# Linear attention ahead of two feed-forward layers: state summed in PSUM, chunks in pairs, 64 by 64 products

## The reference

```python
gamma = 1.0 - 2.0 ** (-5.0 - np.arange(H))          # one decay per head
for t in range(S):
    state = gamma * state + outer(k[:, :, t], v[:, :, t])     # 64 x 64 per head
    y[:, :, t] = scale * (q[:, :, t] @ state)
x = y as (B * S, H * D)                              # 1536 x 512
x = gelu_like(x @ w_in) @ w_out                      # 512 -> 2048 -> 512
x = rms_normalised(x); out = (silu(x @ w_gate) * (x @ w_val)) @ w_out2    # 512 -> 1536 -> 512
```

## Time and profile before

| | us |
|---|---|
| median of 3 runs (586.87 to 587.15) | 587.14 |
| the profiled execution's own time | 587.46 |
| its span, first to last instruction | 585.6 |
| attention: first scores to first product of the layers | 5.46 to 55.26 |
| TensorE busy over the span | 575.1 (98%) |

### The profile page before, as it was taken

One profiled execution on the slowest core, in us unless ns is written; L12 is line 12 of the kernel. 1 busy time (PEld: TensorE's weight loads), 2 busy tenths in 40 slices (PEclk: granted clock), 3 DMA queues, 4 the chain that ended last, 5 costly groups with the idle time before them and its releaser, 6 DMA issues.

```text
span 585.6 us, 9221 instructions
## 1 busy us (share of the span) xinstructions
PE 575.1 (98%) x3558; PEld 552.0 (94%) x3558; DVE 356.0 (61%) x472; ACT 307.8 (53%) x533; POOL 169.2 (29%) x187
## 2 busy tenths in 40 slices
PE   6999999999999999999999999999999999999997
PEld 6888999999999999999999999998889999998886
DVE  3599555667334666876426768668764666667332
ACT  1556666744325766654337655563544555564321
POOL 2674444000122452000123453410060544420000
PEclk8999999999999999999999999999999999999999
DMA  8990122321211222322202222223213322223202
GB/s 324 347 315 29 58 69 72 109 86 59 73 37 36 73 73 72 109 73 72 67 8 72 73 73 73 72 73 108 73 37 103 114 72 73 73 72 109 72 0 107
DMA packets 24363, 52.83 MB, mean 90 GB/s; under 512 B 1920, under 2 KB 2048, under 8 KB 24320
## 3 DMA queue, kind: packets, MB, share of 16 engines
q1 hardware_dynamic: 23744, 50.93, 26.9%
q10 hardware_dynamic: 576, 1.32, 0.6%
HBM read 49.09 MB, written 3.15 MB: 89 GB/s over the span
## 4 chain that ended last, share of the span: by engine, by line
PE 95%; DVE 2%; DMA 2%; issue 1%; SPq 0%; ACT 0%
PE bank L470 39%; PE bank L420 17%; PE bank L422 17%; PE bank L423 17%; DMA arena<-attn_in 2%; PE bank L394 1%; PE bank L363 1%; PE bank L388 1%; DVE arena L823 1%; PE bank L373 1%; DVE arena L841 1%; PE bank L511 0%; DVE x_lo L723 0%; DVE w_lo L714 0%; DVE t L736 0%
## 5 line engine op out<-in xcount | busy, mean ns | idle before, releaser
L420 PE MATMUL bank<-x_hi,w_hi 128*128 128x384 f32 x560 | 187.3, 334 | 0.0
L423 PE MATMUL bank<-x_hi,w_lo 128*128 128x384 f32 x560 | 187.1, 334 | 0.0
L422 PE MATMUL bank<-x_lo,w_hi 128*128 128x384 f32 x560 | 187.1, 334 | 0.0
L714 DVE TENSOR_TENSOR w_lo<-raw,w_hi 128x512 fp32r<-128x512 f32 (+2 forms) x148 | 145.9, 1001 | 50.9 <-ACT w_hi L543 50.7
L975 POOL TENSOR_TENSOR raw<-raw 128x256 f32<-128x256 f32 x40 | 31.9, 796 | 324.1 <-DMA raw<-w 324.1
L543 ACT ACTIVATE w_hi<-raw 128x512 fp32r<-128x512 f32 (+2 forms) x148 | 109.0, 763 | 18.5 <-PE bank L423 10.2
L420 PEld LDWEIGHTS bank<-x_hi,w_hi 128*128 128x128 f32 x560 | 105.1, 188 | 0.1
L422 PEld LDWEIGHTS bank<-x_lo,w_hi 128*128 128x128 f32 x560 | 105.1, 188 | 0.1
L423 PEld LDWEIGHTS bank<-x_hi,w_lo 128*128 128x128 f32 x560 | 105.1, 188 | 0.0
L573 ACT ACTIVATE g_hi<-arena 128x768 fp32r<-128x768 f32 x56 | 47.5, 848 | 103.1 <-PE bank L470 103.1
L749 DVE TENSOR_TENSOR g_lo<-arena,g_hi 128x768 fp32r<-128x768 f32 x56 | 55.2, 986 | 75.2 <-ACT g_hi L573 75.2
(11 more groups left out here) (70 smaller groups left out, 591.0 us busy)
## 6 DMA issues: line engine op xcount, KB each, us to landing
raw<-w SPq DMA_DIRECT2D x68, 512.0 KB, 3.5
arena<-attn_in SPq DMA_DIRECT2D x22, 512.0 KB, 6.7
out<-x SPq DMA_DIRECT2D x1, 1536.0 KB, 7.8
out<-x SPq DMA_DIRECT2D x6, 256.0 KB, 2.0
arena<-attn_in ACTq DMA_DIRECT2D x2, 512.0 KB, 8.1
arena<-tables SPq DMA_DIRECT2D x1, 512.0 KB, 6.7
arena<-tables ACTq DMA_DIRECT2D x1, 256.0 KB, 10.6
ident<-ident_in SPq DMA_DIRECT2D x1, 64.0 KB, 11.4
```

Of the source, the lines that this page charges most:

```text
L420: pe.matmul(dst, w_hi[q][:, w], x_hi[:, x], start=start and kk == 0, stop=False, skip_group_check=True)
L422: pe.matmul(dst, w_hi[q][:, w], x_lo[:, x], start=False, stop=False, skip_group_check=True)
L423: mm = pe.matmul(dst, w_lo[q][:, w], x_hi[:, x], start=False, stop=kk == 1, skip_group_check=True)
L714: dve.tensor_tensor(w_lo[q % 3][:, dst], src, w_hi[q % 3][:, dst].bitcast(F32), ALU.subtract)\
```

## The change

1. **State in PSUM.** The recurrence "new = decay x old + contribution" is replaced by a running sum that is not decayed. The keys of chunk c are scaled by a table of their own, the old one times gamma to the power of -128c (`k_table`); the contributions of a batch are then summed by TensorE in one PSUM bank (`val[g]`, `start` only in chunk 0), and VectorE makes the state from the sum with one multiplication (`g_table`), or a copy for chunk 0. ScalarE's multiplications of the state (line 637) and the semaphore for them are gone.
2. **The tables** are worked out at the start. Two rows of the decay table are fetched by two new transfers, each copied to all 128 partitions (128 x 8 numbers), ahead of ScalarE's other transfers. VectorE multiplies them, GpSimd takes the power -1, VectorE refines it in three instructions, and makes four tables for keys and three for states, each instruction behind the one before it. The masks wait for the last of them.
3. **Compact state.** The state is 128 x 256, the zeros are gone, and so are the two memsets; the cross part is 8 products of 64 by 64 of the array in place of 4 of 128 by 128, both heads of a pair into the same bank, on different partitions.
4. **Pairs of chunks.** TensorE does the scores of two steps, the cross part of two, then contribution, outputs of both, contribution. VectorE, ScalarE, GpSimd and SyncE are ordered to match, and the preparations for the layers lie elsewhere.
5. **One mask instruction.** The PSUM banks of a step's scores are one tensor of 1024 columns (`twin`), multiplied by one instruction.
6. **Transfers.** SyncE loads queries and keys of step 1 ahead of the mask, and the first weights in the first batch of transfers.

Eleven small instructions stand ahead of the first mask, where before there were two memsets. The core of the diff:

```diff
-        state = [part(512) for _ in range(2)]
-        state_dec = [part(512) for _ in range(2)]
+        state = [part(256) for _ in range(2)]
+        k_table = [table[:, T_K:T_K + HEADS]] + [part(HEADS) for _ in range(1, CHUNKS - 1)]
+        g_table = [None, table[:, T_G:T_G + PAIRS]] + [part(PAIRS) for _ in range(2, CHUNKS - 1)]
...
             load(0)
+            load(1)
             sp.dma_start(table[:, T_MASK:T_Q], tables[:, T_MASK:T_Q]).then_inc(mask_in, 16)
-            load(1)
+            load_kv(2)
             load(2)
-            load_kv(2)
             load(3)
             load_kv(3)
+            load_weights(0)
...
+            for a in range(SLOTS, STEPS, 2):
+                for b in (a, a + 1):
+                    sp.wait_ge(scores_done, b - SLOTS + 1)
+                    if (b - SLOTS) % CHUNKS > 0:
+                        sp.wait_ge(q_decayed, cross_at(b - SLOTS) + 1)
+                    load(b)
+                for b in (a, a + 1):
+                    sp.wait_ge(y_done, b - SLOTS + 1)
+                    load_kv(b)
...
+            def new_products(a):
+                r, m = a % SLOTS, state_at(a)
+                g, c = chunk_of(a)
+                if c == CHUNKS - 1:
+                    return
...
+                pe.wait_ge(k_decayed, m + 1)
+                if c > 0:
+                    pe.wait_ge(state_done, m)
+                for p in range(PAIRS):
+                    for h in range(2):
+                        mm = pe.matmul(val[g][64 * h:64 * h + 64, cols(p, 64)],
+                                       k_dec[m % 2][:, cols(2 * p + h, 64)], v[:, cols(2 * p + h, 64)],
+                                       start=c == 0 and p == 0, stop=c == CHUNKS - 2, skip_group_check=True)
+                mm.then_inc(kv_done, 1)
+
+            def from_state(a):
+                par, x = a % 2, cross_at(a)
+                if a >= 2:
+                    pe.wait_ge(y_copied, a - 1)
+                if a % CHUNKS > 0:
+                    pe.wait_ge(q_decayed, x + 1)
+                    pe.wait_ge(state_done, x + 1)
                     for p in range(PAIRS):
-                        mm = pe.matmul(gate[par][:, cols(p, P)], state[x % 2][:, cols(p, P)],
-                                       q_dec[x % 2][:, cols(p, P)], start=p == 0, stop=False, skip_group_check=True)
+                        for h in range(2):
+                            rows = slice(64 * h, 64 * h + 64)
+                            mm = pe.matmul(gate[par][rows, cols(p, P)], state[x % 2][rows, cols(p, 64)],
+                                           q_dec[x % 2][rows, cols(p, P)], start=p == 0, stop=False,
+                                           skip_group_check=True)
                     mm.then_inc(cross_done, 1)
...
+            for a in range(0, STEPS, 2):
+                scores(a)
+                scores(a + 1)
+                if a == 0:
+                    new_products(0)
+                    from_state(0)
+                    from_chunk(0)
+                    from_state(1)
+                    new_products(1)
+                else:
+                    from_state(a)
+                    from_state(a + 1)
+                    new_products(a + 1)
+                    from_chunk(a)
+                from_chunk(a + 1)
+                if a + 2 < STEPS:
+                    new_products(a + 2)
...
+            for k, row in enumerate((first_row, next_row)):
+                at_ = (CHUNK - 2) * k
+                act.dma_start(row, tables[at_:at_ + 1, T_K:T_K + HEADS].to_broadcast([P, HEADS])).then_inc(rows_in, 16)
...
-                if c < CHUNKS - 2:
-                    act.wait_ge(state_done, m + 1)
-                    for p in range(PAIRS):
-                        ins = act.activation(state_dec[m % 2][:, cols(p, P)], state[m % 2][:, cols(p, P)],
-                                             ACT.Copy, scale=table[:, T_G + p:T_G + p + 1])
-                    ins.then_inc(state_decayed, 1)
...
+            dve.wait_ge(rows_in, 32)
+            dve.tensor_tensor(growth, first_row, next_row, ALU.mult).then_inc(decay_set, 1)
+            dve.wait_ge(inverted, 1)
...
+            for c in range(1, CHUNKS - 1):
+                dve.wait_ge(decay_set, c + 3)
+                dve.tensor_tensor(k_table[c], k_table[c - 1], power, ALU.mult).then_inc(decay_set, 1)
+            for c in range(2, CHUNKS - 1):
+                dve.wait_ge(decay_set, c + 6)
+                dve.tensor_tensor(g_table[c], g_table[c - 1], g_table[1], ALU.mult).then_inc(decay_set, 1)
...
+                dve.tensor_tensor(prob[a % 2], twin[a % 2][:, :], table[:, T_MASK:T_Q], ALU.mult)\
+                   .then_inc(probs_done, 1)
...
+                if c == 0:
+                    ins = dve.tensor_copy(state[m % 2], val[g][:, 0:256])
+                else:
+                    new, sums = (t.rearrange("p (k e) -> p k e", k=PAIRS) for t in (state[m % 2], val[g][:, 0:256]))
+                    ins = dve.tensor_tensor(new, sums, g_table[c].unsqueeze(2).to_broadcast([P, PAIRS, 64]), ALU.mult)
...
             dve.wait_ge(mask_in, 16)
+            dve.wait_ge(decay_set, 2 * CHUNKS - 1)
+            for a in range(0, STEPS, 2):
+                masked(a)
+                if a == 0:
+                    new_state(0)
+                masked(a + 1)
                 if a == 4:
                     lower_x(0, B11)
+                elif a == 8:
+                    sum_x(0, T2)
+                new_state(a + 1)
...
+            pool.tensor_tensor(power, growth, minus_one, ALU.pow).then_inc(inverted, 1)
             pool.wait_ge(decay_in, 16)
             decay_k(0)
-            decay_k(1)
             pool.wait_ge(q_table_in, 16)
+            pool.wait_ge(decay_set, 2 * CHUNKS - 1)
+            for a in range(0, STEPS, 2):
+                for b in (a, a + 1):
+                    if b % CHUNKS > 0:
+                        decay_q(b)
+                for b in (a + 1, a + 2):
+                    if b < STEPS and b % CHUNKS < CHUNKS - 1:
+                        decay_k(b)
```

More of the change, by code:

```diff
@@ L100, in transformer_kernel @@
         k_dec = [part(512) for _ in range(2)]
-        state = [part(512) for _ in range(2)]
-        state_dec = [part(512) for _ in range(2)]
+        state = [part(256) for _ in range(2)]
+        k_table = [table[:, T_K:T_K + HEADS]] + [part(HEADS) for _ in range(1, CHUNKS - 1)]
+        g_table = [None, table[:, T_G:T_G + PAIRS]] + [part(PAIRS) for _ in range(2, CHUNKS - 1)]
+        first_row, next_row = part(HEADS), part(HEADS)
+        growth, rest, power = part(HEADS), part(HEADS), part(HEADS)
+        minus_one = part(HEADS)
         used[0] = 0
@@ L107, in transformer_kernel @@
         m5 = [part(HALF) for _ in range(2)]
-        bank = [ctx.enter_context(nc.psum_tensor(f"bank{i}", [P, 512], F32)) for i in range(8)]
+        twin = [ctx.enter_context(nc.psum_tensor(f"twin{i}", [P, 1024], F32)) for i in range(2)]
+        bank = [twin[i // 2][:, 512 * (i % 2):512 * (i % 2) + 512] for i in range(4)]
+        bank += [ctx.enter_context(nc.psum_tensor(f"bank{i}", [P, 512], F32)) for i in range(4, 8)]
         acc, gate, val = bank[0:4], bank[4:6], bank[6:8]
@@ L352, in _, with scores @@
         def _(pe):
[L354 to L356 removed]
+            def scores(a):
+                par, r = a % 2, a % SLOTS
+                q, k = slot[r][:, 0:512], slot[r][:, 512:1024]
                 pe.wait_ge(qk_in[r], 16 * (a // SLOTS) + 16)
                 if a >= 2:
[L359 removed]
+                    pe.wait_ge(probs_done, a - 1)
                 for p in range(PAIRS):
@@ L396, in outputs @@
                                        prob[par][:, 512 * h + P * p:512 * h + P * p + P],
-                                       start=not cross and p == 0, stop=True, skip_group_check=True)
+                                       start=a % CHUNKS == 0 and p == 0, stop=True, skip_group_check=True)
                 mm.then_inc(y_done, 1)
@@ L625, in _, with copy_y @@
             act.wait_ge(decay_in, 16)
-            for a in range(STEPS):
-                par, m = a % 2, state_at(a)
+            def copy_y(a):
                 g, c = chunk_of(a)
@@ L832, in new_state @@
                     dve.wait_ge(cross_done, m - 1)
-                if c > 0:
-                    dve.wait_ge(state_decayed, (CHUNKS - 2) * g + c)
-                for h in range(2):
-                    rows = slice(64 * h, 64 * h + 64)
-                    new, old = (t[m_ % 2][rows, :].rearrange("p (k e) -> p k e", k=PAIRS)[:, :, 64 * h:64 * h + 64]
-                                for t, m_ in ((state, m), (state_dec, m - 1)))
-                    kv = val[m % 2][rows, 0:256].rearrange("p (k e) -> p k e", k=PAIRS)
-                    if c > 0:
-                        ins = dve.tensor_tensor(new, kv, old, ALU.add)
-                    else:
-                        ins = dve.tensor_copy(new, kv)
+                if c == 0:
[3 more added lines that the diff above has]
```

(1 more changed line is left out.)

125 lines of the change are left out of this document (50 added, 75 removed).

## The result

| | before | changed |
|---|---|---|
| median, us | 587.14 | 590.22 (589.81 to 590.75) |
| profiled execution's own time, span | 587.46, 585.6 | 590.75, 589.0 |
| ratio of the runs | | 1.0043, 95% interval 1.0028 to 1.0058 |
| first product of the layers | 55.26 | 57.39 |

Forecast were 585.2 and 581.8 to 588.2. In the profile the attention ends 2.1 us later than before, where I had it 1.9 us earlier, and 1.3 more are lost behind it: from the layers' first product to the end it is 531.6 us and was 530.3.

The account below looks back on a forecast made before the run. TensorE, busy 98% of the span, was taken as the bound; -3.9 us of shapes, -2.7 of waits and +4.7 at the start took the median from 587.14 to 585.2 us, range 581.8 to 588.2.

Parts of the forecast that it names:

- Tile shapes, -3.9 us: TensorE in the attention: groups of one kind side by side pay for fewer tile-shape changes, saving 3.9 us.
- 64 by 64 products, zero: Cross part: the two heads' products run side by side at the old pace, no gain and no loss.
- The small transfers, +4.4 us: Start, ScalarE's queue: two transfers of 128 small pieces delay what stands behind them by 2.2 us each, 4.4 together.
- the pace in the sum: Start: a small packet costs its queue a large one's time, queues taking turns; 117 packets in some 2.3 us.
- The 0.2 us worked out: Start: the skill page's 10.5 ns per small packet would have both small transfers gone in 0.2 us; not adopted.
- The half clock, 0 to 1.5, taken 0.5: Start: TensorE, mostly idle from 8.7 to 18, runs partly at 1.2 GHz, costing 0 to 1.5 us, 0.5 taken.
- Nothing, with the same cover: Slots in the pairs: step a+4's keys and values, needed 6.8 less 1.2 us after request, land in time; no cost.
- What is late next ... 2 us of slack: VectorE: pair 10's mask comes up to 0.5 us late behind pair 8's extras, but its output has 2 us slack.
- The waits of before, -2.7: Middle of the attention: TensorE's 2.7 us of waits, chiefly for states VectorE made late, go with the sum in PSUM.
- rival D: Slower: query table past 20 us, or middle pairs each waiting some tenths for GpSimd; 588 to 590, chance 0.08.
- the forecast 31.65 us of the pairs: TensorE's time for the five pairs from step 2 on, up to the layers: 31.65 us, including 2.75 for shapes.

Follow-up runs that it names:

- y2: y1 with TensorE's order alone changed to scores(a), cross(a), scores(a+1), cross(a+1) in pairs 2, 4, 8 and 10; 586.59 us, ratio 0.9963.
- x1: The kernel before with only the two small transfers added ahead of ScalarE's others, into a buffer nobody reads; 591.65 us, ratio 1.0055.
- z3: The changed kernel itself, unmodified, measured again in 9 runs beside the kernel before; 590.12 us, ratio 1.0032.
- x3: The changed kernel with 24 products of ones keeping TensorE busy in two waits of the start; 588.42 us, ratio 0.9999.
- x4: The changed kernel with six slots instead of four, so keys and values are asked for two outputs earlier; 588.09 us, ratio 0.9995.
- y1: The changed kernel without the small transfers and the power (factor by memsets), and with six slots; 585.14 us, ratio 0.9938.
- y4: The changed kernel with only VectorE's preparations reordered as in y3; ratio 1.0003.
- y3: y1 with VectorE's preparations for the layers in another order; 583.66 us, ratio 0.9917.
- z2: y3 with the mask moved ahead of step 1's queries and keys, the query table ahead of its keys and values; 582.80 us, ratio 0.9909.
- z1: y3 with 5 and 6 products of ones in TensorE's two waits of the start; 582.97 us, ratio 0.9913.

## Why the prediction was wrong, step by step

- **Tile shapes, -3.9 us: right.** The steps inside groups and at joins came as read: a pair without a wait takes 6.71 us where two steps took 7.64, and y2 shows the price by itself, 0.17 a change where 0.20 was read.
- **64 by 64 products, zero: right.** Two cross groups take 1.90 us from start to start, 0.11 a pair. The Trainium skill's sentence ("TensorEngine Tiling (Array Packing)", "Restrictions and Gotchas") that row tiles cannot access one PSUM bank at once did not hold for tiles on different partitions of the bank; here the measurement decides.
- **The small transfers, +4.4 us: right in size, the mechanism only in part.** The changed kernel has 3.7 at the keys and at the query, x1 4.1, and x1 alone costs 3.2 us of time, more than the whole forecast gain. They hold back their queue, as forecast. But the pace in the sum (117 small packets in 2.3 us) did not come: from 2.0 to 4.5 us there were 61, and the other queue was slow too, which taking turns does not explain; that the sum came out close is in part luck. The 0.2 us worked out with the figure of the Trainium skill ("DMA: Bandwidth & Descriptors", section "Measured (HBM→SBUF, 128 partitions, SWDGE, issued from GpSimd)") divides by 16 once too often: its 10.5 ns a packet come from 0.67 us for 64 packets, so 256 are 2.7 us, an estimate by that page.
- **The half clock, 0 to 1.5, taken 0.5: mis-sized.** It cost 2.7 in the profile (cross part to scores of step 2: 5.5 us, at full clock 3.0 in z3; and 0.2 in those scores), and 1.9 to 2.6 by the ratios of x3 and the changed kernel. It alone made the scores of step 2 late, by 1.6 in all, since the cross part before them came 0.3 early. I had taken the stretch of before as the longest possible, though I had myself worked out that TensorE would be idle for longer.
- **"Nothing, with the same cover", transfers and GpSimd: failed, 2.2 us.** I wrote that keys of step a+4 are needed 5.6 us after they are asked for and "land in time". They took 5.8 (29.01 to 34.78), and GpSimd then needed 1.66, not 1.15. The means in the earlier trace rows hid that the two engines are slow in the same moments. The cover was not the same: before, 8.0 us lay between the request and TensorE's use and 6.3 were needed; now there are 7.1, and 7.4 are needed. x4 gives 1.1 to 2.0 us back, y1 less. How much of it is the transfer and how much GpSimd beside VectorE is not parted: no run has the one without the other.
- **"What is late next ... 2 us of slack": failed, 1.3 us.** I followed VectorE's queue to the masks of the last pair but not to the sum of quadrants behind them, on which ScalarE's first copy of the layers hangs. y4 shows it: 531.6 us behind the first product become 530.4.
- **The waits of before, -2.7: right**, they are gone, but others took their place. That was the second half of rival D (waits for GpSimd in the pairs), which I gave 0.08 and priced at 588 to 590. It came together with the clock and with the stall behind the pairs; 590.2 is the sum of three misses in one direction.

What stays open: why single packets of the transfers from 27 to 35 us took up to 2 us. Over that stretch the packets of SyncE's queue filled 80.6% of the 16 engines' time, so the queue was not free; and 5.3 us for the same keys in the kernel before say that 5.8 is little out of the way. Six slots hid it in x4 and not in y1; its cause was not tried. No run reached the forecast 31.65 us of the pairs; the nearest, y3 and z2, have 32.5. The 64 by 64 shape was not undone alone, since the rows left nothing to ask.

## What to carry to other kernels

Look at a small transfer's packets and at what stands behind it in its queue, not only at its bytes: 8 KB in 256 packets ahead of the first inputs cost 3.2 us. Put products of one tile shape side by side, 0.15 to 0.20 us for each change saved here. And when work is paired or batched, ask of each buffer how much time is now left between its release and its next use; the gain on the busiest engine was real here and was lost to that, to the small transfers, to the half clock and to the order of a second engine. With the transfers gone, six slots and the other order, the same change is 0.8 to 0.9% faster than the kernel before.

## What the runs showed that I had not expected

- The stretch at half clock differs between executions of one kernel with one start: 10.2 and 3.4 us in two profiles of the changed kernel, 6.8 and none in y3 and y1, whose starts are the same. The executions differ by 1.2 to 1.4 us accordingly. Only the kernels that kept TensorE busy (x3, z1) were free of it, or nearly (0.999), in every run.
- Two transfers that each copy 32 bytes to 128 partitions slowed the other queue too: from 2.0 to 4.5 us SyncE's queue moved 83 packets in the changed kernel, 86 in x1 and 147 before.
- VectorE and GpSimd working side by side on 768 and 512 columns took 1.80 and 1.66 us where each alone took 0.96 and 1.04. No run tried it by itself.
